# Hand-over of a routed MLP: the last group's list positions ahead of its row scaling, and two small TensorE steps a quarter of a tile later

## What is computed

```
kv  = einsum('bhsd,bhse->bhde', k, v);  a = einsum('bhsd,bhde->bhse', q, kv)
x   = rms_normalise(a) * g_norm, rearranged to (4608 tokens, 512)
x   = relu(x @ w_in)**2 @ w_out                         # 512 -> 2048 -> 512
e   = argmax(x @ w_gate + modality_bias[modality_id])   # 8 experts
out = softmax weight of e * (relu(x @ w1[e]) @ w2[e])   # 512 -> 1024 -> 512
```

## Time and profile before

| | |
|---|---|
| median of 3 runs | 1402.18 us (1401.32 to 1407.2) |
| the profiled execution | 1402.4 us, of which the span from first to last instruction is 1400.5 us |
| PE busy | 1371.1 us, 98% of the span |
| DVE, ACT, POOL busy | 57%, 42%, 36% |
| mean granted TensorE clock | 0.996 of full speed |

### The profile page before, as it was taken

The page is one execution under the profiler, slowest core; times in us unless marked ns, Lnnn a source line. Parts: engine busy times, 40 slices in busy tenths (PEclk is TensorE's granted clock), DMA queues, the critical chain, the costliest instruction groups (busy, mean ns, idle before and its releaser), DMA issues. The chain is left out here.

```text
span 1400.5 us, 20900 instructions
## 1 busy us (share of the span) xinstructions
PE 1371.1 (98%) x7063; PEld 1112.8 (79%) x7063; DVE 791.9 (57%) x1677; ACT 591.6 (42%) x1201; POOL 498.1 (36%) x589
## 2 busy tenths in 40 slices
PE   5999999999999999999999999998999999999998
PEld 5788888888888888887888887876788878888876
DVE  3456474474574573574574655546555555555555
ACT  3443334234233243333333343334555555555553
POOL 2643232232232132132132134504555555555551
PEclk9999999999999999999999999999999999999999
DMA  9634547557556556567474464778995113851270
GB/s 236 168 106 154 184 126 195 185 122 204 172 132 198 175 126 207 171 123 222 155 147 155 149 151 148 203 264 200 349 356 193 47 47 113 301 203 47 67 263 20
DMA packets 178917, 237.45 MB, mean 170 GB/s; under 512 B 57838, under 2 KB 97166, under 8 KB 178834
## 3 DMA queue, kind: packets, MB, share of 16 engines
q1 hardware_dynamic: 164530, 214.84, 51.9%
q0 software_dynamic: 9472, 19.96, 4.4%
q10 hardware_dynamic: 4832, 1.57, 0.6%
HBM read 148.07 MB, written 89.30 MB: 169 GB/s over the span
## 5 line engine op out<-in xcount | busy, mean ns | idle before, releaser
L664 POOL TENSOR_TENSOR stage<-stage,stage_hi 128x512 f32<-128x512 f32 x128 | 169.2, 1322 | 558.8 <-ACT stage_hi L1142 558.6
L1478 DVE TENSOR_TENSOR g_sb<-g_sb 128x512 f32<-128x512 f32 x144 | 102.1, 709 | 328.0 <-ACT g_hi L1206 323.3
L1204 ACT ACTIVATE g_sb<-ps_h 128x512 f32<-128x512 f32 x144 | 85.9, 596 | 436.5 <-DVE g_lo L1482 242.2
L809 PE MATMUL ps_h<-xT_hi,weights 128*128 128x512 f32 (+1 forms) x580 | 232.1, 400 | 0.0
L809 PE MATMUL ps_y<-g_hi,weights 128*128 128x512 f32 x576 | 231.6, 402 | 0.0
L811 PE MATMUL ps_h<-xT_hi,weights 128*128 128x512 f32 (+1 forms) x580 | 225.9, 390 | 0.0
L810 PE MATMUL ps_h<-xT_lo,weights 128*128 128x512 f32 (+1 forms) x580 | 225.3, 388 | 0.0
L811 PE MATMUL ps_y<-g_hi,weights 128*128 128x512 f32 x576 | 224.9, 390 | 0.0
L810 PE MATMUL ps_y<-g_lo,weights 128*128 128x512 f32 x576 | 224.7, 390 | 0.0
L1232 ACT ACTIVATE kv_sb<-ps_h 32x256 f32<-32x256 f32 x456 | 170.7, 374 | 122.2 <-PE ps_h L994 116.9
L994 PE MATMUL ps_y<-weights,xT_hi 128*128 128x512 f32 x656 | 177.1, 392 | 0.5 <-DVE xT_lo L1659 0.5
(11 more groups left out here) (267 smaller groups left out, 1744.9 us busy)
## 6 DMA issues: line engine op xcount, KB each, us to landing
stage<-in_moe_w SPq DMA_DIRECT2D x128, 256.0 KB
w_hi<-stage_hi SPq DMA_DIRECT2D x128, 256.0 KB
w_lo<-stage SPq DMA_DIRECT2D x128, 256.0 KB
weights<-w_hi SPq DMA_DIRECT2D x32, 1024.0 KB
weights<-w_lo SPq DMA_DIRECT2D x32, 1024.0 KB
rows<-y_sb SPq DMA_DIRECT2D x36, 256.0 KB
k_sb<-in_k SPq DMA_DIRECT2D x30, 288.0 KB, 4.6
v_sb<-in_v SPq DMA_DIRECT2D x30, 288.0 KB, 5.4
```

What stands on the lines that cost most here:

```text
L664: pool.tensor_tensor(stage[n % 2][:, :], stage[n % 2][:, :], stage_hi[n % 2][:, :].bitcast(F32), ALU.subtract).then_inc(split_lo, 1)
L809: pe.matmul(out_ap, lhs[0], rhs[0], start=start, stop=False)
L1204: act.activation(g_sb[:, :], ps_h[c % 2][:, 0:GROUP], ACT.Relu).then_inc(h_read, 1)
L1478: dve.tensor_tensor(g_sb[:, :], g_sb[:, :], g_sb[:, :], ALU.mult).then_inc(g_done, 1)
```

## The change

On DVE the seven small instructions of the last group's list positions go ahead of the four scalings of its rows; the slot comparisons stay behind both. On PE the 12 slot products go from the end of hidden(1), ahead of output(0), to a place inside output(0), behind its first six instructions ("quarter of output"). The four spreading products that use their result go from that place to the middle of output(0), behind twelve.

```diff
                 elif place == "hidden":
                     pe.wait_ge(entries_done, GROUPS)
                     pe.matmul(ps_b[0:1, 0:E], ones[:, 0:1], before[:, 0, :], start=True, stop=True).then_inc(counts_ps, 1)
+
+            def third_places(place):
+
+                if place == "quarter of output":
                     pe.wait_ge(slots_done, TILES + 1)
                     for b in range(SLOT_BLOCKS):
                         for t in range(TILES):
                             last = pe.matmul(ps_slot_ids[:, b:b + 1], slot_of[t][:, b * P:(b + 1) * P], sent_past[:, t:t + 1],
                                              start=(t == 0), stop=(t == TILES - 1))
                     last.then_inc(slot_ids_ps, 1)
-
-            def third_places(place):
-
-                if place == "quarter of output":
+                elif place == "middle":
                     pe.wait_ge(ids_in_block_done, 2)
                     for b in range(4):
                         last = pe.matmul(ps_next[b * QUAD:(b + 1) * QUAD, :], of_strips[:, :],
...
             routing("argmax", last_group)
             routing("gate", last_group)
             take_gates(last_group)
+            routing("prefix", last_group)
             for k_ in range(KC):
                 scale_rows(last_group, k_, y_turned_last)
-            routing("prefix", last_group)
             find_slots()
             turn_h(0, 0)
             turn_h(0, 1)
```

## The result

The changed kernel takes 1408.23 us (median of 17 runs, 1406.58 to 1410.92); beside it the kernel before took 1402.56 us (17 runs, 1400.57 to 1407.2). The ratio is 1.0034, 95% interval 1.0028 to 1.0041, so 4.8 us slower (3.9 to 5.7); the two medians by themselves differ by 5.7. That is less than the 0.5% set as a bound, but outside the predicted range of 1400.0 to 1406.4 and 3.7 us or more over the forecast of 1403.2. The profiled execution took 1406.94 us, of which the span is 1405.0.

The account below looks back on a forecast made before the run. PE, busy 98% of the span, was taken as the bound. POOL's copy 2.7 us later, less 1.7 of room, cost 1.0 at hidden(3): 1403.2 us on the median of 1402.18, range 1400.0 to 1406.4.

Parts of the forecast that it names:

- The gap: PE ahead of output(0): idles from 947.44 to 950.85, 3.41 us instead of 1.35.
- The queues' starts: POOL's scatters start 2.42 us earlier, SP's row stores 1.48 later; the lists are read 2.4 earlier.
- The price of a narrow product: Slot products on PE: 0.21 us each at half clock against 0.1125 at full, taken from the transposes at 28.6 us.
- The clock: PE in output(0): half clock from 951.5 to 955.0, as in the earlier trace, so output(0) ends at 960.9.
- the copy: POOL's copy of tile 3's addresses: starts at 962.0, 2.7 us later, held by `tiles_done` at 960.5 plus 1.5.
- my slower rival: Half clock through all slot products: they end at 959.0, hidden(3) starts 3.4 us later, 1405.6 us; chance 0.16.
- PE's own way: PE's work up to hidden(3) without waiting for tile 3's rows: hidden(3) could start at 973.1.
- The register reading: POOL between `tiles_done` and copying tile 3's addresses: 1.5 us, bounds 0 and 3.77.
- The landing: Tile 3's rows, from the last fetch's issue until they are in: 3.6 us, between 3.0 and 4.2.
- The later rows alone would make it 1.48 later, so they are covered: POOL's copy of tile 3's addresses: later stored rows delay it 1.48 us, less than the 2.7 from late `tiles_done`.
- forecast at tile 3: Start of hidden(3), the mark: set by tile 3's rows at 975.0 against 974.02 before, 1.0 us lost.
- a start of tile 3 later by x makes the end later by x: Steady tiles: PE has no gap from 1008 to 1385 us, so a shift of their start moves the end equally.

Follow-up runs that it names:

- e13: The changed kernel with expert 1's later weight loads put behind the lists and tile 3's rows, and 14 full-width dummy products in PE's gap; ratio to before 1.0008.
- e10: The changed kernel with expert 1's later first weights and second weights put behind the lists and tile 3's rows; ratio to before 1.0045.
- e5: The changed kernel with expert 1's second weights held on SP until both halves of tile 3's rows are in; ratio to before 1.0035.
- e1: The kernel before with DVE's reorder alone, list positions ahead of row scaling, PE's order as before; ratio to before 1.0038.
- e4: The changed kernel with DVE's count of tiles ahead of the slot numbers instead of behind them; ratio to before 1.0028.
- e2: The changed kernel with DVE's old order, so PE's moves alone; ratio to before 1.0048.
- e6: The kernel before with DVE's reorder alone, plus expert 1's second weights held until tile 3's rows are in; ratio to before 1.0019.
- e9: The kernel before with DVE's reorder, and expert 1's later weight loads put behind the lists and tile 3's rows; ratio to before 1.0015.
- e3: The changed kernel with 14 full-width dummy products in PE's gap ahead of output(0); ratio to before 1.0033.
- e11: The changed kernel with 14 dummy products in PE's gap, the count of tiles first, and expert 1's second weights held until tile 3's rows landed; ratio 1.0018.
- e14: The kernel before with expert 1's later weight loads put behind the lists and tile 3's rows, and five dummy products in PE's 1.35 us gap; ratio 0.9997.
- e7: The kernel before with expert 1's later first weights and second weights put behind the lists and tile 3's rows; 1404.3 us against 1402.93, ratio 1.0013.
- e8: The kernel before with DVE's reorder, and POOL's scatters of the positions held until the rows are scaled; ratio to before 1.0029.
- e12: The changed kernel with 14 dummy products, the count of tiles first, and expert 1's later weight loads put behind tile 3's rows; ratio 1.0010.

## Why the prediction was wrong

The two parts of the chain that I took from rows of before and that don't touch the clock or DMA traffic hold within 0.3 us. Distances are again from the gates' copy.

- **The gap, right.** Forecast 3.41 us, measured 3.33, and output(0) starts at 7.62 (forecast 950.85, which is 7.73).
- **The queues' starts, right.** Scatters 2.53 earlier (forecast 2.42), row stores 1.37 later (1.48). The lists are read at 19.19 instead of 23.45, 4.3 earlier where I had taken 2.4; nobody waits for them any more, as forecast.
- **The price of a narrow product, right.** 24 in 4.97 us, 0.21 each, against 0.11 in e13 at full clock. The row of transposes that I took it from the earlier trace rows was a good one. The Trainium skill, page "TensorE: Matmul & The Clock Gate", section "LDWEIGHTS (loading the stationary operand)", gives columns divided by 1.2 ns without regard to the clock, which makes 107 ns for 128 columns, an estimate. That agrees with the full clock here and not with the half one.
- **The clock, wrong, and this is the first failed step.** I wrote "With half clock from 951.5 to 955, as in the trace", and so had the clock come back in the middle of the slot products. It fell at 950.3 and stayed at half until 963.9. In the kernel before, the full-width products of output(0) followed the fall; here 24 narrow ones did. The slot products ended at 15.29 behind the gates' copy and not at 13.5, `tiles_done` came at 19.2 and not 17.4, the copy at 20.77 and not 18.9. This was my slower rival (`tiles_done` 962.9, copy 964.4, here 962.3 and 963.9 on before's clock), to which I gave 0.16. e13 against e10 shows that the clock is worth 3.22 us at tile 3.
- **PE's own way, wrong by the same step.** I had it at 973.1, which is 29.98, and so 1.9 short of tile 3's rows. Measured, without the wait of 1.53, it is 33.98: the slot products ended 1.8 later than forecast, and the 18 wide and 8 small products behind them took 6.61 us instead of 4.31, as the clock was still at half. Even my slower rival had it at 975.5, here 977.1, because it let the clock come back right behind the slot products. So 3.1 of the 4.6 us were lost on PE alone, and no earlier fetch could have saved them; e5 and e10, in which the rows are in time, show tile 3 at 33.0.
- **The register reading, right.** 1.55 us (forecast 1.5).
- **The landing, wrong, the second failed step.** "In this place it was at most 4.16 [...] I take 3.6", with 4.2 as the upper bound. It was 4.83, and up to 5.9 in e1 to e4. The bound was misread too: 4.16 ran to the turn of the first half (971.03), and to that of the last it was 4.54. SP issues expert 1's second weights when the lists are in, and I never set their start against the fetch. Before it lay 3.2 us behind the fetch's last issue, in the changed kernel 3.9 ahead. Two things did that: the lists came earlier, and the fetch came 4.8 later. In e1 it takes the earlier lists (weights at 24.28, last issue ended at 26.75); in e2 the later fetch alone does it (26.56 and 27.77). e5 and e6, with the weights held, land in up to 3.0 and in 1.9.
- **"The later rows alone would make it 1.48 later, so they are covered", wrong in size, third.** With the weights in the queue it is 3.0 (e1), without them 1.36 (e9). It was covered in the changed kernel, by 1.5 us only (rows at 19.2 to 19.4 in the other kernels, the copy at 20.77), and it is one reason why e3 and e4 gained so little; the late landing is the other.

The sum: forecast at tile 3 is 975.0 − 943.12 = 31.88, measured 35.51. The copy gives 1.87 of the difference, its chain to the last fetch 0.2, the landing 1.2, and the way from landing to start 0.3, which makes 3.6. Added to the forecast of 1403.2 that gives 1406.8, and 1402.18 x 1.0034 is 1406.9. The slower rival had the first term and not the landing, so even it stopped at 1405.6. The range ended at 1406.4 because I had put the landing bound at 4.2 (1405.6 + 0.6 is 1406.2; I had set it 0.2 wider). The four terms say where tile 3's rows were late. Had the last two been as forecast, tile 3 would still have stood at PE's own way, 33.98 in this profile and 33.0 in e5, above the forecast's 31.88.

That a start of tile 3 later by x makes the end later by x held in the changed kernel (4.61 at tile 3, 4.12 at tile 6, 3.5 at the end of this profile, 4.8 by the ratio). It does not hold for kernels that move the weights: in e5, e6, e9, e11 and e14 one to four us won at tile 3 were given back by tile 6, or at expert 1. e11 is the plainest: tile 3 is 0.28 later than before, tile 6 is 3.9.

Left open: why 2 MB of weights behind the rows cost 0 to 0.4 us in the order of before (16.18 against 16.23 in e14 and 15.77 in e7) and 2.1 in the new one (19.22 against 17.13). e8 excludes only that the scatters go first. Open too is how the clock decides, and why in one and the same order of PE it falls up to 2.8 us earlier in one profile than in another; I tell only what preceded each fall and rise. And how often the changed kernel's runs have the 13.5 us of its profile, and how often the 10 us of e2, e4, e5 and e10, no run here shows.

## What to carry to other kernels

Narrow products moved behind a gap of PE were run at half clock here, and the clock stayed down over them and behind them. Take the fall that the trace shows for a case with wide work behind it as the lower bound, price the wide work behind the narrow products at half clock too, and put the work that another engine waits for ahead of the gap, or fill the gap. Look at the clock in more than one profile before you compare two of them. When a step is made earlier, or another later, ask what is queued behind it on the same queue, and what that will now meet. Where two chains end within 1 to 2 us of each other, mend both in one experiment, or each will seem to be worth little.

## What the runs showed of the hardware

- A fetch of 128 rows in two halves landed in 1.7 to 2.1 us where SP's loads had not started (e6, e9, e11, e14) or started only 0.1 us ahead of the last issue's end (e8), and in 4.8 to 5.9 us when SP had started two 1 MB loads 1.2 to 3.9 us ahead of it (the change, e1 to e4). The other profiles name no wait.
- With 2 MB of loads behind it on the same queue, a 1 MB store landed 2.1 us later than without them (e1 against e9; 19.2 to 19.4 in six profiles against 17.0 to 17.2 in three), though they were issued after it. In the order of before it was 0 to 0.4.
- At half clock also a product of a single column, with its weight load of 128 columns, takes double, 0.21 against 0.11 us (the change against e13).
- With 3.3 us of idling, six wide products and then the one-column work, the granted clock was at half for 10 us (e2, e4, e5, e10) or 13.5 (the change), though PE's records show it busy for 8.00 of 8.00 us in the middle of that. With 3.5 us of products of full width in the gap it stayed full over the one-column work, and fell for 3.5 us only 0.3 to 1.2 us behind it (e11, e12, e13) or not at all (e3).
- In one order of PE the clock's fall came at different places in different profiles, 6.2 to 8.8 us behind the copy of the gates (before, e1, e6 to e9), and lasted 3.5 or 7 us.
